# Transformer chain on one core: scores in two pairs of banks, a first batch without value differences, and a reordered weight fold

## What is computed

```python
# stage 1: attention, 8 heads of 64, window of 128 tokens, ALiBi bias
scores = scale * q @ k.T + bias ; masked where not 0 <= rel < 128
x = softmax(scores) @ v                      # -> (B, 576, 512)
# stage 2: gated unit with a spatial product
h = relu(x @ w_in) ; u, v = h[..., :512], h[..., 512:]
v_n = (v - mean) / sqrt(var + 1e-6)
g = u * (w_spatial @ v_n + b_spatial) ; y = g @ w_out
# stage 3: 4 causal attention experts of width 64, the top 2 of 4 mixed by a softmax of y @ w_gate
out = sum_e weight_e * (softmax(causal(y wq_e (y wk_e).T)) @ (y wv_e) @ wo_e)
```

## Time and profile before

| | us |
|---|---|
| median of the timed runs | 496.91 (495.17 to 497.12, 3 runs) |
| the profiled execution | 496.05 |
| its span, first to last instruction | 494.2 |
| PE busy | 474.0 |
| DVE busy | 320.9 |
| ACT busy | 271.7 |
| POOL busy | 213.6 |

### The profile page before, as it was taken

One profiled execution on the slowest core, in us unless ns is written; L12 is line 12 of the kernel. 1 busy time (PEld: TensorE's weight loads), 2 busy tenths in 40 slices (PEclk: granted clock), 3 DMA queues, 4 the chain that ended last, 5 costly groups with the idle time before them and its releaser, 6 DMA issues.

```text
span 494.2 us, 10632 instructions
## 1 busy us (share of the span) xinstructions
PE 474.0 (96%) x3794; PEld 404.1 (82%) x3794; DVE 320.9 (65%) x1247; ACT 271.7 (55%) x822; POOL 213.6 (43%) x378
## 2 busy tenths in 40 slices
PE   8689989999999999999999999999999999999996
PEld 5457989899776789999776779999876779999874
DVE  6886875257778855437778865436777975335783
ACT  5667563246676744235666654335666663335663
POOL 4494628222344526742253525760443442461431
PEclk9999999999999999999999999999999999999999
DMA  7927520003201073002311063001311000000111
GB/s 235 320 55 217 201 86 0 1 2 76 91 22 44 2 197 91 1 1 48 109 34 44 1 184 106 0 2 40 95 44 56 1 1 2 0 2 8 42 43 54
DMA packets 33512, 31.64 MB, mean 64 GB/s; under 512 B 6002, under 2 KB 24434, under 8 KB 33460
## 3 DMA queue, kind: packets, MB, share of 16 engines
q1 hardware_dynamic: 33460, 30.97, 20.6%
HBM read 23.88 MB, written 4.72 MB: 58 GB/s over the span
## 4 chain that ended last, share of the span: by engine, by line
PE 73%; DVE 14%; ACT 7%; issue 3%; POOL 2%; DVEq 0%; POOLq 0%
PE bank L1385 16%; PE bank L1387 15%; PE bank L1386 15%; PE bank L1372 6%; PE bank L1450 6%; ACT p L825 4%; PE bank L1412 3%; DVE ring L936 3%; PE bank L1614 3%; PE bank L1629 2%; PE bank L1651 2%; DVE p L1170 2%; PE bank L1391 2%; PE bank L1392 1%; POOL ring L542 1%
## 5 line engine op out<-in xcount | busy, mean ns | idle before, releaser
L542 POOL TENSOR_SCALAR ring<-ring,r 128x128 f32<-128x128 f32 x144 | 62.4, 447 | 80.1 <-DVE r L956 79.8
L628 POOL TENSOR_SCALAR p<-p,r,wgt 128x128 f32<-128x128 f32 (+3 forms) x64 | 38.6, 616 | 92.9 <-DVE wgt_last L1217 49.9
L656 ACT ACTIVATE ring<-ring,neg 128x128 f32<-128x128 f32 x144 | 56.7, 396 | 23.9 <-DVE ring L947 19.4
L825 ACT ACTIVATE p<-p,neg 128x128 f32<-128x128 f32 (+4 forms) x72 | 41.7, 580 | 31.9 <-DVE neg L1170 31.9
L936 DVE CUSTOM_DVE_ANT_0 ring<-bank,bias 128x256 f32<-128x256 f32 (+1 forms) x128 | 43.7, 385 | 6.1 <-PE bank L1372 5.6
L1372 PE MATMUL bank<-k,q 64*128 64x256 f32 (+2 forms) x320 | 39.0, 372 | 2.8 <-DVE neg L936 2.8
L592 POOL TENSOR_TENSOR g_lo<-uT,g_hi 128x288 fp32r<-128x288 f32 x32 | 26.8, 862 | 32.1 <-ACT g_hi L791 32.1
L1385 PE MATMUL bank<-g_hi,w_c_hi 128*128 128x288 f32 x128 | 38.3, 299 | 2.1 <-DVE k_lo L1273 2.1
L1385 PE MATMUL bank<-w_spatial_hi,vn_hi 128*128 128x288 f32 x128 | 37.9, 296 | 2.3 <-DVE uT L1149 2.3
L1385 PE MATMUL bank<-x_hi,w_in_hi 128*128 128x288 f32 x128 | 38.2, 298 | 0.0
L1387 PE MATMUL bank<-x_hi,w_in_lo 128*128 128x288 f32 x128 | 37.7, 294 | 0.0
(11 more groups left out here) (193 smaller groups left out, 1447.7 us busy)
## 6 DMA issues: line engine op xcount, KB each, us to landing
v_in<-v SPq DMA_DIRECT2D x16, 256.0 KB, 3.9
out<-o_sb SPq DMA_DIRECT2D x16, 256.0 KB, 2.0
q<-qT SPq DMA_DIRECT2D x15, 256.0 KB, 4.5
k<-kT SPq DMA_DIRECT2D x15, 256.0 KB, 4.8
v_minus_v_of_tile_above<-v SPq DMA_DIRECT2D x9, 256.0 KB, 3.9
w_in_raw<-w_in SPq DMA_DIRECT2D x4, 512.0 KB, 5.7
w_cat_raw<-wcat SPq DMA_DIRECT2D x1, 1544.0 KB, 7.1
w_spatial_raw<-wsT SPq DMA_DIRECT2D x1, 1152.0 KB, 8.6
```

The source lines that it names most:

```text
L542: last = nc.gpsimd.tensor_scalar(p, p, r1[:, i % 2, h:h + 1], 0.0, ALU.mult, ALU.add)
L628: nc.gpsimd.tensor_scalar(p, p, r3[:, i % 2, e:e + 1], by, ALU.mult, ALU.mult).then_inc(s3_sd, 1)
L656: nc.scalar.activation(x, x, ACT.Exp, bias=neg1[:, u % SLOTS1:u % SLOTS1 + 1], scale=-1.0, accum_out=sum1[:, i % 2, h:h + 1]).then_inc(s1_ ...
L825: nc.scalar.activation(p, p, ACT.Exp, bias=neg3[:, w % 4:w % 4 + 1], scale=-1.0, accum_out=sum3[:, i % 2, es[0]:es[0] + 1]).then_inc(s3_ex, 1)
```

## The change

- **Banks of the scores.** Steps four and six of stage 1 write banks 3 and 6 instead of 0 and 1. The scores of steps four and five are issued together in step two (behind its transposes), those of six and seven together at the head of step four; before, each of these was issued one or two steps ahead on its own. A step's scores now wait for the bias of the step before the last. In later batches step four also waits until the last output of the batch before has been copied from bank 6. All transposes of blocks one to four go to bank 2.
- **Values of the first batch.** POOL's differences are gone. ACT negates v of four blocks (`negate_v`, steps one, three, five and seven), and PE adds a product with v of the block itself. The zero rows for the last block are written to `v_in`.
- **Mask table.** ACT writes its zeros before the first exponential, not POOL in step three.
- **Fold.** ACT takes w_out before the v columns of w_cat. DVE does two low parts ahead of the multiplications with u and the other ten between the second four of these. PE waits for the low parts as it needs them. POOL waits for all twelve before its subtractions of stage 2.
- **Stage 3.** `high_qk(4)` and `low_qk(4)` move ahead of two exponentials and of one reciprocal; `high_z(0)` moves ahead of the exponential of group nine.
- **Start of later batches.** DVE's `join1` of group five moves behind `copy_pt1_second(0)`, and both ahead of the reciprocal of group three.

```diff
+SECOND_BANKS_AT = (4, 6)
-            return (6, 7) if b == 0 and m == 1 else S1_BANKS
+            return (6, 7) if b == 0 and m == 1 else (3, 6) if m in SECOND_BANKS_AT else S1_BANKS
-            return 2 + (g % 2 if G1[g][0] == 0 else g // 2 % 2)
+            return 2 + (g % 2 if G1[g][0] == 0 else 0)
...
-                    link(nc.gpsimd.memset(masks[:], 0.0))
+                    pool.wait_ge(s_mz, 1)
...
-                nc.gpsimd.tensor_tensor(v_step[0:r, t - 1], v_in[0:r, t], v_in[0:r, t - 1], ALU.subtract).then_inc(s_vd, 1)
...
+                if first:
+                    pool.wait_ge(s_fsl, 3 * KT)
                 for i in range(8):
...
+            nc.scalar.copy(masks[:].rearrange("p (a c) -> p a c", c=LAST),
+                           pt_hi[:, 0, 0:LAST].bitcast(F32).unsqueeze(1).to_broadcast([P, 1024 // LAST + 1, LAST])).then_inc(s_mz, 1)
...
+                def negate_v(t):
+                    act.wait_ge(s_v_in[t], 16)
+                    nc.scalar.activation(v_step[:, t], v_in[:, t], ACT.Copy, scale=-1.0).then_inc(s_vneg, 1)
...
+                    if first and m % 2 and m < ND1 - 1:
+                        negate_v(m // 2)
...
+                high_qk(4)
                 exp3(0)
                 exp3(1)
-                high_qk(4)
...
+                        if w == 2 * E + 1:
+                            high_z(0)
                         exp3(w)
...
                     if m == 0 and not first:
+                        copy_pt1_second(0)
+                        join1(b, 5)
                         reciprocal1(b, 3)
-                    if m == 0 and not first:
-                        copy_pt1_second(0)
                         reciprocal1(b, 4)
...
                 if first:
+                    low_w_qk(0)
+                    low_w_qk(1)
                 for i in range(8):
...
+                    if first and i == 4:
+                        low_w_qk(2)
+                        low_w_qk(3)
+                        low_w_outT(0)
+                    if first and i == 5:
+                        low_w_outT(1)
+                        low_w_outT(2)
+                    if first and i == 6:
+                        low_w_outT(3)
+                        low_w_v(0)
+                    if first and i == 7:
+                        low_w_v(1)
+                        low_w_v(2)
...
+                low_qk(4)
                 reciprocal3(0)
-                low_qk(4)
...
-                if m:
+                if m == 4 and b:
+                    pe.wait_ge(s3_o, NT * b)
+                elif m in (4, 5, 6, 7):
+                    pe.wait_ge(s1_bi, U1 * b + units1(2 * m - (4 if m == 4 else 2))[0][0])
+                elif m:
...
                     for d in range(KT):
+                        if j == 0:
+                            pe.wait_ge(s_fsl, KT + d + 1)
...
+                        if first:
+                            product(g, v_in[:, qb], 1, False, False)
                         product(g, v_step[:, qb - 1], 1, False, True)
...
-                    if (3 <= m or (m == 0 and first)) and m + AHEAD1 < ND1 - 1:
-                        scores1(b, m + AHEAD1)
-                        if m + AHEAD1 == ND1 - 2:
-                            scores1(b, ND1 - 1)
+                    if m == 0 and first:
+                        scores1(b, 2)
+                    if m in (4, 6):
+                        scores1(b, m + 2)
+                        scores1(b, m + 3)
                     transpose1(b, 2 * m)
                     transpose1(b, 2 * m + 1)
...
-                    if 1 <= m <= 2:
-                        scores1(b, m + AHEAD1)
+                    if m == 1:
+                        scores1(b, 3)
+                    if m == 2:
+                        scores1(b, 4)
+                        scores1(b, 5)
```

More of the change, by code:

```diff
@@ L849, in row @@
                         nc.scalar.copy(wcat_qk_hi[:, d, :], wcat_raw[:, d, 0:CUT]).then_inc(s_fsh, 1)
+                    act.wait_ge(s_woT, 16)
+                    for d in range(KT):
+                        nc.scalar.copy(woT_hi[:, d, :], woT_raw[:, d, :]).then_inc(s_fsh, 1)
                     act.wait_ge(s1_vll, 1)
@@ L852, in row @@
                         nc.scalar.copy(wcat_v_hi[:, d, :], wcat_raw[:, d, CUT:CW]).then_inc(s_fsh, 1)
-                    act.wait_ge(s_woT, 16)
-                    for d in range(KT):
-                        nc.scalar.copy(woT_hi[:, d, :], woT_raw[:, d, :]).then_inc(s_fsh, 1)
                 for i in range(8):
@@ L890, in row @@
                 for m in range(ND3):
-                    for i in range(NT - 2):
+                    for i in range(1, NT - 2):
                         if m == DEND3[i] + 1:
@@ L1151, in row @@
                 if first:
+                    low_w_v(3)
                     for j, (t, c0, c1) in enumerate(FOLD):
```

46 lines of the change are left out of this document (22 added, 24 removed).

## The result

The median went from 496.76 us (495.17 to 497.12, four runs) to 489.30 us (488.56 to 489.65, four runs): a ratio of 0.9854 with a 95% interval of 0.983 to 0.9878, or 7.5 us less. The forecast was 491.9 by a sum of -4.6; the time lies in its range, and the change is faster, as forecast. It does not lie in the forecast's own narrower range of 490.3 to 493.8, and it is nearer to rival (1), 488.2, than to the forecast. The sum was too small by a third: the profiled executions differ by 6.8 us.

The account below looks back on a forecast made before the run. PE's own list was taken as the bound, except in the opening and at recurring waits for one engine. Terms -2.1 - 1.3 - 1.8 + 0.6 = -4.6 us, from 496.5, gave 491.9 us; range 488.3 to 495.6.

Parts of the forecast that it names:

- rival (1): DVE's chain is looser than read: stage 3 gives 3.4 us, later batches 0.5 each; 488.2 us in all; chance 0.17.
- The fold, -2.1: At the fifth spatial piece, PE's 2.28 us wait for DVE's multiplication with u goes; 2.1 us less, ends -2.3 and -1.0.
- The opening, -1.3: First batch's start: added products cost 3.1 us, regained idle time gives 4.4; ends -2.6 and +1.2.
- The 4.4 regained: In the opening, PE gets back 4.4 of about 5.7 us of idle time that can be had.
- 6.1 us of work between scalings for which PE waits: In the opening, POOL loses four differences of 1.27 us and the mask's zeros of 1.00 us.
- On the shared path of DVE and POOL: In the opening, each difference taken from POOL frees at most 1.27 us of DVE; the sum does not use it.
- Stage 3, four times, -1.8: Waits for k's low part and split output go; about half of 3.4 us returns, 0.45 a batch; ends -3.4 and 0.
- Stage 1 of the later batches, +0.6: Later three batches lose 0.2 us each: PE meets DVE's full list later, and the batch start delays POOL's scaling.
- Rival 2: The opening does not pay for its products: only two POOL waits, 1.9 us, come back; 494.4 us; chance 0.18.
- Rival 3: Waits move on to PE's next places: the fold gives 1.0 us, all else cancels; 495.5 us; chance 0.12.
- Rival 4: Grouped scores in steps two and four hold transposes back, 1.1 us each; slower by 3.6, 500.1 us; chance 0.06.
- What was to show it: Signs: fold, split-output and opening POOL-scaling waits gone; first stage 1 shorter by 1 to 2 us, later batches by about 0.3.

## Why the prediction was right, and where it was not

- **The bound.** Right: PE's list, except in the opening and at recurring places where it waits for one turn of one engine. Every gain found was such a wait.
- **The fold, -2.1.** Right in mechanism, small by 0.4: it measured 2.5. The late low parts did not come in (PE has no wait in the fold), and the 0.2 us that came back beside the wait was no term of the sum; what it is isn't shown. What was named as late next, DVE, was not late.
- **The opening, -1.3.** The sum was met (-1.19 in the profiled executions; -1.15 from the first transposes on, at the full clock) by luck: its terms were not. The 3.1 for sixteen products were right. The 4.4 regained I put mostly on POOL's freed time; measured, the change of the values with its products is worth about nothing without the pairs (40.69 against 40.76), with the pairs it costs 0.2 to 0.7 us (39.44 against 39.61 and 40.17, a comparison that the falls of the clock blur), and beside idle products and early reciprocals it gains 0.56. The pairs of scores are worth 1.1 us. The failed step is "6.1 us of work between scalings for which PE waits": the first difference lies in a pause in which POOL waits for DVE's reciprocal, and only the difference and the tables between 24 and 36 us were in PE's way, where the two waits of 1.9 us are gone. PE still waits for POOL at two places in step three:

```profile
17.85 0.44 PE L1441 MATMUL bank<-ident,ring 128*128 128x128 f32 x2 [0.37 <-POOL ring L539]
...
19.23 0.44 PE L1441 MATMUL bank<-ident,ring 128*128 128x128 f32 x2 [0.94 <-POOL ring L539]
```

- **On the shared path of DVE and POOL** the trace had the join of 1.05 us beside POOL's subtraction, and the Trainium skill (SBUF — State Buffer, section "Who interferes with whom") gave that its reason. The traces with the values as before agree once more, and in both orders: beside POOL's fourth difference the mask product took 1.80 us, or the difference 1.79, whichever began second. By that rule the opening should have moved towards -2.6. It did not, as a lost 0.6 us has a price only where PE waits for it: PE waited for the mask product in one kernel (0.83 us), and for POOL's difference in none.
- **Stage 3, four times, -1.8.** The step that failed in size. The two waits were named and went, but "I expect about half" was a guess without a row. It measured 3.0 (3.05 in the marks after the change, 3.02 by the edit that puts it back), nine tenths of the 3.4 of the waits. What I feared for, low part, top two and next maxima 0.2 us later, had slack, which the profile could have told me: no wait of PE for any of them was among those that I read.
- **Stage 1 of the later batches, +0.6.** Measured 0.00, +0.03 and +0.02. The reading of the earlier trace rows, that DVE's list is full and a wait removed from PE comes back further on, was right and is shown by the shortened joins. The price set on it (0.3 for the join's new place, and more for scores ahead of transposes) was not: the place of the join is worth 0.04 to 0.09 us and the pairs 0.1 us the other way.
- **The rivals.** Rival 1, a looser DVE, was right for stage 3 (3.0 of its 3.4) and wrong for the later batches (0 instead of -1.5). Its two halves should have been two rivals, since the slack of different places decides them. Rival 2 had its argument right, that the new products don't pay by themselves, but the opening was paid by the pairs. Rival 3 is seen in stage 1 of later batches, and in the opening in part: the waits for POOL in step three are new. Rival 4 needed 0.65 us a group; the pairs gained 0.1.
- **What was to show it.** Seen: no wait for u's multiplication, no split output in the list, an end of the first batch's stage 1 that is 1.19 us sooner, a wait for POOL's scaling in place of the one ahead of step four's scores. Not seen: an opening without waits for POOL; and a later batch is shorter by 0.77 us (113.93 to 113.16 between first transposes), not by 0.3, which is the third stage again.
- **From trace to median.** The profiled executions give 6.8 us, the medians 7.5. The fold's wait can carry a fall of the clock with it, at 1.5 us, and that is gone with it. The repeated runs of the kernel before don't settle whether this is the 0.7: the three with a mean clock of 0.999 or more took 495.7 to 495.8 us, but the eighteen with less took 495.2 to 497.5, some of them less than those three. The cause of the 0.7 stays open.
- **Slips.** The 7.93 us of the opening are 39% of PE's idle time, not nearly half. The ends of the range, 488.3 and 495.6, stand 0.1 above what rivals (1) and (3) sum to.

With the measured terms the sum is -2.5 - 1.15 - 3.05 + 0 = -6.7. The last product of the changed kernel's second execution, 7.53 us sooner than in the first of the kernel before, is this and 0.83 us of an earlier start.

## What to carry to other kernels

A wait of the bounding engine on a chain that is late by one misplaced instruction (here two exponentials, six low parts) came back almost whole when the instruction was moved, as none of those moved behind it was then waited for; discount it by a row, not by a habit. A wait at which the engine waited for was itself without idle time mostly moved on when the order changed; less work there shortened it. Work moved off an engine was worth nothing where that engine spent the freed time waiting, and something where it had no pause: look at what stands before each piece of it before its duration is put into a sum.

## What the runs showed of the hardware

- After the fold's wait of 2.27 to 2.28 us TensorE's granted clock stayed at 1.00 in one execution of the kernel before and fell to 0.79 in the mean of a stretch of 4 us in the other. In the changed kernel it fell to 0.57 behind waits of 0.37, 0.94 and 0.96 us in one execution and not in the other. The same program and the same waits: which execution has it is chance, and it is worth 1.5 and 0.5 us. A later fall in the same opening (0.73 and 0.84 at 20 to 24 and 24 to 28 us, in the kernel with short joins) made the opening 40.55 us, 0.9 more than without one.
- The start differs by chance as well: the first transposes began at 9.35 and 8.99 us in the two executions of the kernel before, at 8.75 and 8.52 in those of the changed one, and at 8.98 with its waits and reciprocals edited. PE's idle products ahead of them, in the kernel before and after:

```profile
6.71 1.65 PE L1381 MATMUL bank<-pt_hi 128*128 128x512 f32 x4
```

```profile
7.12 0.63 PE L1408 MATMUL bank<-pt_hi 128*128 128x512 f32 x2
```

  The four start 0.43 us apart, the two 0.23. That is the spacing of the two levels of the clock, but the profile's granted clock is 1.00 at 4 to 8 us in both, so the clock isn't shown to be the cause. The first 0.60 of the 1.19 us of the opening need not be the change's.
- Two groups of scores in a row take less than two apart: by the distance of starts 1.93 us for 16 records (the next product starts at 151.96), against 1.07 for 8 apart, so up to 0.21 us less for a pair.

```profile
150.03 2.00 PE L1399 MATMUL bank<-k,q 64*128 64x256 f32 x16
```

- DVE and POOL can hold each other up: a mask product of DVE that takes 0.69 us took 1.80 beside a subtraction of POOL that began 0.03 us before it, and where the mask product began 0.03 us before, the subtraction took 1.79 instead of 1.27.
